# One level of Strassen for h, on 512-token blocks, with W_out streamed from DRAM

## What is computed

```python
scores = np.where(block_i >= block_j, q @ k.T / 8, -1e9)
x = softmax(scores) @ v                     # heads side by side: (2304, 512)
h = x @ moe_w_in                            # (2304, 2048)
x = (h * np.clip(h + 3.0, 0.0, 6.0) / 6.0) @ moe_w_out
h = x @ moe2_w_in
out = (h * np.tanh(np.log1p(np.exp(h)))) @ moe2_w_out
```

## Time and profile before

| what | us |
|---|---|
| median of 3 runs (lowest, highest) | 1022.93 (1021.42, 1024.57) |
| the profiled execution, whole | 1022.14 |
| its span, first to last instruction | 1020.3 |
| PE busy in the span | 995.0 |
| DVE, ACT, POOL busy | 662.3, 530.9, 279.7 |
| DMA moved | 78.89 MB, 77 GB/s over the span |

### The profile page before, as it was taken

How to read it: one execution, slowest core, us unless ns; L and a number is a source line. 1 busy time by engine, 2 the same in 40 slices (tenths; PEclk the granted TensorE clock), 3 DMA queues, 4 the chain that set the end, 5 groups by cost and what they waited for, 6 DMA issues and landing times.

```text
span 1020.3 us, 16901 instructions
## 1 busy us (share of the span) xinstructions
PE 995.0 (98%) x5700; PEld 931.1 (91%) x5700; DVE 662.3 (65%) x1280; ACT 530.9 (52%) x1161; POOL 279.7 (27%) x296
## 2 busy tenths in 40 slices
PE   6999999989999999999999999999999999999998
PEld 5888888889999999999999999999999999999996
DVE  5889889857332222222323559978888888888876
ACT  6889889846232222232323546555555465555553
POOL 7889889926022031130210200101001000010000
PEclk9999999989999999999999999999999999999999
DMA  6877886448121020120200342001000010000000
GB/s 156 238 184 212 212 208 169 101 142 257 39 73 52 20 81 23 54 69 0 88 28 31 132 140 75 24 1 48 16 31 23 8 39 23 0 31 0 32 1 31
DMA packets 42261, 78.89 MB, mean 77 GB/s; under 512 B 8032, under 2 KB 27616, under 8 KB 42208
## 3 DMA queue, kind: packets, MB, share of 16 engines
q1 hardware_dynamic: 36080, 68.48, 23.8%
q10 hardware_dynamic: 6128, 9.73, 2.6%
HBM read 59.24 MB, written 18.95 MB: 77 GB/s over the span
## 4 chain that ended last, share of the span: by engine, by line
PE 90%; DVE 4%; POOL 2%; issue 2%; ACT 1%; DMA 1%; SPq 0%; DVEq 0%; POOLq 0%
PE psum L525 38%; PE psum L500 13%; PE psum L502 13%; PE psum L501 13%; PE psum L451 4%; PE psum L430 4%; PE psum L406 3%; PE psum L411 3%; DMA qkin<-in_qk 0%; PE psum L409 0%; ACT prob L599 0%; POOL xraw L1002 0%; POOL xlo L1008 0%; DVE gsplit L845 0%; DVE wlo_early L832 0%
## 5 line engine op out<-in xcount | busy, mean ns | idle before, releaser
L1008 POOL TENSOR_TENSOR xlo<-xraw,xhi 128x384 f32 (+1 forms) x48 | 58.4, 1220 | 599.5 <-ACT xhi L659 599.5
L878 DVE SCALAR_TENSOR_TENSOR gbuf<-ebuf,psum 128x384 f32<-128x384 f32 x96 | 53.0, 552 | 218.3 <-ACT ebuf L711 218.3
L711 ACT ACTIVATE ebuf<-psum,three 128x384 f32<-128x384 f32 x96 | 55.7, 581 | 241.9 <-PE psum L502 241.9
L500 PE MATMUL psum<-xhi,whi_early 128*128 (+1 forms) x384 | 129.7, 338 | 1.3 <-POOL xlo L1008 1.3
L502 PE MATMUL psum<-xhi,wlo_early 128*128 (+1 forms) x384 | 129.4, 337 | 0.0
L501 PE MATMUL psum<-xlo,whi_early 128*128 (+1 forms) x384 | 129.2, 337 | 0.0
L502 PE MATMUL psum<-xhi,wlo_late 128*128 (+1 forms) x384 | 129.0, 336 | 0.0
L500 PE MATMUL psum<-xhi,whi_late 128*128 (+1 forms) x384 | 128.9, 336 | 0.0
L501 PE MATMUL psum<-xlo,whi_late 128*128 (+1 forms) x384 | 128.7, 335 | 0.0
L684 ACT ACTIVATE gsplit<-gbuf 128x384 fp32r<-128x384 f32 x192 | 100.1, 521 | 54.9 <-DVE gbuf L899 53.4
L845 DVE SCALAR_TENSOR_TENSOR gsplit<-gbuf,gsplit 128x384 fp32r<-128x384 f32 x192 | 123.0, 640 | 4.2 <-ACT gsplit L684 3.5
(11 more groups left out here) (89 smaller groups left out, 2298.2 us busy)
## 6 DMA issues: line engine op xcount, KB each, us to landing
wraw<-in_w SPq DMA_DIRECT2D x32, 512.0 KB, 3.5
qkin<-in_qk SPq DMA_DIRECT2D x43, 288.0 KB, 4.4
xraw<-attn_t SPq DMA_DIRECT2D x24, 384.0 KB, 3.3
attn_t<-late SPq DMA_DIRECT2D x44, 144.0 KB, 3.2
ystage<-in_qk SPq DMA_DIRECT2D x20, 288.0 KB, 4.5
xraw<-r_d SPq DMA_DIRECT2D x48, 96.0 KB, 3.3
x_t<-ystage ACTq DMA_DIRECT2D x24, 192.0 KB, 1.9
xraw<-x_t SPq DMA_DIRECT2D x24, 192.0 KB, 2.4
```

Source lines behind the costliest of these rows:

```text
L500: pe.matmul(bank(f % HB, TB), hi, x_part(xhi, blk, c), start=(c == 0), stop=False)
L711: nc.scalar.activation(ebuf[f % 2][:, :], bank(f % HB, TB), ACT.Relu, bias=three[:, 0:1]).then_inc(act_ready, 1)
L878: nc.vector.scalar_tensor_tensor(out=gbuf[f % 2][:, :], in0=e, scalar=6.0, in1=h, op0=ALU.min, op1=ALU.mult).then_inc(g_ready, 1)
L1008: nc.gpsimd.tensor_tensor(x_part(xlo, blk, c), xraw[c][:, 0, :], x_part(xhi, blk, c).bitcast(F32), ALU.subtract).then_inc(x_lo, 1)
```

## The change

**h by Strassen.** Blocks of tokens are now `plain` (256 tokens, the first of each layer) or full (512 tokens, four in each layer). The hidden dimension goes in 8 pairs of f; a `step` g is one pair in one block, 40 for each layer, 80 in all. For a full block, W_in's 512 x 256 piece and x's 512 x 512 block are cut in quarters, and the four quarters of h are made from 7 products instead of 8, in Winograd's form: with S1 = A21 + A22, S2 = S1 - A11, S3 = A11 - A21, S4 = A12 - S2 on the weights (DVE, `mix_w`) and T1 to T4 on x (POOL, `mix_x`). Each product is 2 chunks x 3 passes of 256 columns, in PSUM banks x, y, z. Sums that several quarters share are gathered in one bank and copied out on the way by ACT (`snap5`, `snap0`, `snap2`, `snap_3`); DVE adds the rest (`add_c11`, `add_c12`, `add_c22`). M4 may only start after snap3, M7 after snap2, M6 after snap0. For a plain block h stays an ordinary product, 24 matmuls of 256 columns for a pair.

**Order of PE.** The products of step s + 2 stand between the pieces of y of step s, one product and one piece in turn (`h_at`, `y_group`). In the full blocks of layer 0 y has 512 columns, not 384.

**Memory.** W_in's quarters A11, A12, A22 and S1 stay in SBUF (`whi`, `wlo`). S2 to S4 are split, stored to DRAM (`ext_d`, 0.79 MB a pair) and loaded again for each step of a full block (`ext`, two buffers). W_out is split f by f into one of `GS` = 3 slots (`osplit`) in the plain block, stored to `o_d` (`keep_o`, 0.52 MB an f), and loaded from there in the full blocks (`stream_o`). A slot may be filled anew when y of the f three before is done and its store has landed. In layer 0's plain block ACT makes the high part, in layer 1's POOL makes both. In layer 0 the weights of W_in are loaded twice, once for the quarters and once for S2 to S4 (`JOBS`), in steps -1 to 11; in layer 1 once, in steps 31 to 38. Loading, storing and y's stores are all in SP's queue.

**Mish.** e = exp(h), q = min((e + 1)^2, cap) + 1, r = exp(-ln q), and tanh(softplus(h)) = 1 - 2r. ACT makes the square; r gets one step of Newton's rule as before, folded into fewer products (`times_r`, `better_r`, `mish_times_h`).

The diff, cut:

```diff
-TB = 384
-NB = TOK // TB
+SQUARE_CAP = float(2 ** 28)
+TB = 512
+HT = TB // 2
+PAIRS = FT // 2
+NBL = 1 + (TOK - HT) // TB
+GS = 3
+PRODUCT_AT = {0: M2, 1: M5, 2: M1, 3: M3, 4: M6, 6: M7, 8: M4}
+JOBS = ([(0, p, True, False) for p in range(PAIRS)] + [(0, p, False, True) for p in range(PAIRS)] +
+        [(1, p, True, True) for p in range(PAIRS)])
...
@@ SP, after the attention
+            for s in range(-1, STEPS):
...
+                if s + 3 < STEPS and not plain((s + 3) // PAIRS):
+                    load_ext(s + 3)
+                if s > 0 and s % PAIRS == 0:
+                    store_y(s // PAIRS - 1)
+                if job_at(s + 1) is not None:
+                    load_w(job_at(s + 1))
+                if 0 <= s and 2 * s + 2 < 2 * STEPS and streamed(2 * s + 2):
+                    stream_o(2 * s + 2)
+                if 2 * s + 5 < 2 * STEPS and not streamed(2 * s + 5):
+                    load_o(2 * s + 5)
+                for i in (2 * s, 2 * s + 1):
+                    if i >= 0 and not streamed(i):
+                        keep_o(i)
+                blk = (s + 1) // PAIRS + 1
+                if (s + 1) % PAIRS == 0 and blk < NBLK:
+                    load_x(blk, 0)
+                blk = s // PAIRS + 1
+                if s % PAIRS == 2 and blk < NBLK and not plain(blk):
+                    load_x(blk, 1)
+                if 2 * s + 6 < 2 * STEPS and not streamed(2 * s + 6):
+                    load_o(2 * s + 6)
+                if 0 <= s and 2 * s + 3 < 2 * STEPS and streamed(2 * s + 3):
+                    stream_o(2 * s + 3)
+                if job_at(s) is not None and JOBS[job_at(s)][3]:
+                    store_ext(job_at(s))
...
@@ PE
...
+                    pe.wait_ge(snapped, SNAPS[g] + SNAP3 + 1)
+                    accumulate(x_bank(g), *resident(g, A22), g, T4, False, True).then_inc(product, 1)
+            for s in range(STEPS):
+                for k in range(9):
+                    if s + 2 < STEPS:
+                        h_at(s + 2, k)
+                    if k < 8:
+                        y_group(s, k)
...
@@ ACT
+            def split_o_hi(i):
+                act.wait_ge(o_loaded[i % GS], 16 * (i // GS + 1))
+                act.wait_ge(y_step, y_done(i - GS))
+                act.wait_ge(o_kept[i % GS], 16 * kept_before(i, i % GS))
+                nc.scalar.activation(osplit[i % GS][:, 0:D], oraw[i % GS][:, :], ACT.Copy).then_inc(first_o_hi, 1)
+            def mish_period(s):
...
+                    square(s + 1, 0)
+                    activate_h(s + 1, 1)
+                    square(s + 1, 1)
+                    split_g_hi(s, 1)
+                    snap5(s + 2)
+                    ln_d(s + 1, 0)
+                    snap0(s + 2)
+                    ln_d(s + 1, 1)
+                    exp_minus_ln(s + 1, 0)
+                    exp_minus_ln(s + 1, 1)
+                    snap2(s + 2)
+                next_x_hi(s, 0)
+                    activate_h(s + 2, 0)
+                    split_g_hi(s + 1, 0)
+                    snap_3(s + 2)
+                next_x_hi(s, 1)
...
@@ DVE
+            def mish_period(s):
...
+                    cap_square(s + 1, 0)
+                    mish_times_h(s, 1)
+                    cap_square(s + 1, 1)
+                    split_g_lo(s, 1)
+                    add_c11(s + 2)
+                    times_r(s + 1, 0)
+                    better_r(s + 1, 0)
+                    times_r(s + 1, 1)
+                    add_c12(s + 2)
+                    mish_times_h(s + 1, 0)
+                    better_r(s + 1, 1)
+                    split_g_lo(s + 1, 0)
+                    add_c22(s + 2)
...
@@ POOL
+            for s in range(-1, STEPS):
+                if GS <= 2 * s + 2 < 2 * STEPS and not streamed(2 * s + 2):
+                    split_o(2 * s + 2)
+                next_x(s)
+                if GS <= 2 * s + 3 < 2 * STEPS and not streamed(2 * s + 3):
+                    split_o(2 * s + 3)
```

1143 lines of the change are left out of this document (746 added, 397 removed).

## The result

The changed kernel took 1152.15 us in the median of 4 runs (1144.64 to 1157.62), the kernel before 1023.13 beside it (1021.42 to 1024.57): ratio 1.126, with a 95% interval of 1.119 to 1.132. Slower was forecast, but by 33 us and not by 129. The profiled execution has a span of 1149.5 us.

What follows compares the result with a forecast made beforehand. PE, busy 98% of the span, was taken as the bound. 1022.1 - 36.3 (PE) + 42 + 12 + 4 (transfers) + 8 (mish order) + 3 (tail) + 1 (attention) = 1056 us; range 1018 to 1092.

Steps and rivals of the forecast that it cites:

- layer 0's start: Layer 0's first steps: transfers and waits for W_out's slots, x and S2 to S4 cost +42 us (26 to 54).
- The short block of layer 1: Layer 1's first block: the slot loop of store, POOL's copy and subtraction, and load costs +12 us (4 to 20).
- PE's gain: Dense products on PE: h as 3072 matmuls of 256 columns at 118.4 ns; PE alone -36.3 us.
- rival (4): h on PE: a 256-column matmul costs 133 ns, so the gain is gone; 1100 us, chance 0.05.
- Layer 0's relu steps: Layer 0's full steps: ACT has 5.1 of 10.5 us, so they cost nothing.
- x's load: Layer 0's full blocks: the next x's second half stands before a stream PE wants, +4 us (0 to 8).
- (1): Transfers in layer 0's start and the short blocks: they hide, steps 0 to 12 lose 5 us; 1005 us, chance 0.13.
- (2): Layer 0's start: only the bound of 26 us holds, with smaller terms in layer 1; 1025 us, chance 0.11.
- sign for a wrong rate: First 130 us of the dense stage: a DMA rate over 360 GB/s would show the forecast wrong.
- The mish order: Layer 1's full steps: M4 waits 0.1 to 0.35 us for snap3 in each of 32 steps, +8 us (0 to 20).
- Rival (3): Layer 1's full steps: the mish chain closes on itself, steps take 11.5 us, 32 more; 1080 us, chance 0.14.
- The tail: The kernel's end: no h is left to cover the last pair's mish chain, so y(79) waits, +3 us.

Runs made afterwards that it cites:

- e1: The changed kernel with ACT's snap0 ahead of the high half of g for the step's second f in relu steps: 1141.55 us.
- e5: e1 with layer 1's weight splits moved behind the third snapshot and activation on ACT, and behind the last add on DVE: 1120.14 us.
- e6: The changed kernel with the load of x's second half behind W_out's second stream on SP, and x's work behind the second W_out split on POOL: 1173.01 us.
- e8: The changed kernel with the edits of e5, e6 and e7 together: 1093.89 us, ratio 1.067.
- e2: The changed kernel without the stores of split W_out, except the first f of each layer; loads keep number and size: 1132.86 us.
- e7: The changed kernel with each store of split W_out issued a step earlier, right behind the load that waits for the same low half: 1140.83 us.
- e15: e8 with W_out's low halves on DVE in layer 0's short block, and block 1's sum and scaling of x on only 8 columns: 1087.79 us.
- e9: e8 without the stores of split weights, except the first of each kind in each layer; loads keep number and size: 1072.92 us.
- e11: e8 with six extra additions on POOL, for which nobody waits, in each of steps 49 to 77: 1192.88 us.
- e10: e8 with POOL splitting only 64 of 512 columns of each W_out block in layer 1's short block: 1085.33 us.

## Why the prediction was wrong, step by step

Two steps of the sum failed most. The term for the order of ACT and DVE in layer 0's full steps was put at nothing: they lost 57 us, not 4. And layer 0's start was put at 42 us and lost 75. The short block of layer 1 added 17 to its 12.

**PE's gain: right.** The start-to-start distance of h's matmuls, profile after:

```profile
950.00 0.28 PE L703 MATMUL psum<-xhi,whi 128*128 128x256 f32 x1
950.12 0.28 PE L704 MATMUL psum<-xlo,whi 128*128 128x256 f32 x1
950.24 0.28 PE L705 MATMUL psum<-xhi,wlo 128*128 128x256 f32 x1
```

0.12 us, where 0.1184 was taken from the earlier trace rows; steps of 10.55, 8.40, 5.76 where nothing waits. So the -36.3 us are there to within 5 us, and rival (4) is out. (The lower bound of 27 doesn't follow from the rates named: 120 ns gives 33.)

**Layer 0's relu steps: the step that failed.** "Layer 0's relu steps have ACT at 5.1 of 10.5 and cost nothing" judged ACT by its sum. I walked the order for the mish (+8) and not for the relu, where one waiting split stands ahead of a snapshot. It cost 1.32 us in each full step that had nothing else (11.87 against 10.55); e1 gave 18.5 us back in steps 12 to 37. The same sentence named the weight splits as a risk and took them for covered: e5 gave back 11.1 more. x's load, forecast at 4, was 7.1 (e6). These three make 36.7 of the 57 us, and e8 has just these less (330.4 - 293.7). The other 20.7 are still in e8: 11 in steps 31 to 37, where M4 waits for `snap_3`; 6 in steps 12, 19 and 27, from waits of 1.0 to 4.2 us for a stream of `osplit` and the lower clock behind the longest; and 2.6 in steps 13, 21 and 29, where PE waits for x's low half, one of POOL's. The profile after has the same wait:

```profile
409.63 0.39 PE L703 MATMUL psum<-xhi,whi 128*128 128x256 f32 x1 [0.58 <-POOL xlo L1508]
```

No run tried these three.

**The start of layer 0: mechanism partly right, size wrong** (42 forecast, 75 measured). PE waits 6.4 us for `snap0` in steps 6 to 11 as well, but there e1 gave back nothing: another wait took its place. Right: the slots' loop (e2, e7), x ahead of splits in step 4. Wrong: the landings. I took 1.9 us of latency round the moving time, from a transfer alone. DMA issues of the profile after, from 218 to 386 us:

```profile
o_d<-osplit SPq DMA_DIRECT2D x16, 512.0 KB, 7.6
...
osplit<-o_d SPq DMA_DIRECT2D x10, 512.0 KB, 6.8
```

7.6 and 6.8 us in the median for 0.52 MB, against the 3.5 that the walk was built on (5.8 and 5.0 over the whole kernel). And x's first half was not in the walk as a transfer that POOL waits for in step 1, only in step 4: 18 us of idle POOL, then 5.1 of sums, then y's low half. Rivals (1) and (2) are out with 75. The rate was not what failed. A full queue moved 318 and 336 GB/s over 11 to 12 us in e15, and more in short stretches of the profile after, where PE had no work at all:

```profile
290.00:294.00 4.00, 0.00 (x0) 0.00 (x0) 0.43 (x2) 1.45 (x4) 0.75 (x1) 0.50 1.03 423
```

From 332 to 340 us it was 386. So the forecast's sign for a wrong rate, over 360, was there for some microseconds, and 346 was no ceiling. But from 225 to 386 us only 247 moved on average, since engines and queue waited for each other. A bound by bytes and a walk by latencies, each alone, were both too low. (The 42 were called the middle of 26 and 54, which is 40.)

**The clock: not in the sum at all.** Windows and PE's timeline, profile after:

```profile
230.00:238.00 8.00, 0.00 (x0) 0.02 (x1) 1.72 (x3) 2.89 (x6) 6.55 (x6) 0.54 0.62 234
238.00:242.00 4.00, 3.99 (x22) 4.00 (x23) 4.00 (x5) 1.60 (x4) 4.00 (x4) 0.63 0.80 225
```

```profile
269.33 0.55 PE L797 MATMUL psum<-ghi,osplit 128*128 128x256 f32 x1 [6.08 <-POOL osplit L1523]
...
270.75 0.41 PE L703 MATMUL psum<-xhi,whi 128*128 128x256 f32 x1
270.96 0.41 PE L704 MATMUL psum<-xlo,whi 128*128 128x256 f32 x1
271.17 0.41 PE L705 MATMUL psum<-xhi,wlo 128*128 128x256 f32 x1
```

The granted clock was at the lower level (1.2 GHz; 0.50 to 0.63 in these windows), and matmuls of 256 columns came 0.21 us apart instead of 0.12. The same is seen behind seven gaps of PE in steps 1 to 11, the shortest 3.0 us long and the longest 10.5. From 225 to 386 us some 100 distances lie at 0.19 to 0.225 us, and a few of 512 columns at 0.43 instead of 0.23: 11 us of PE in all. From 716 to 811 us it is some 40 and 15, 7 us. So such a gap of PE costs more than its length. Some of that PE time stands before a wait that would have been there anyway, so 11 us is a ceiling for what it added to the start.

**Layer 1's short block: mechanism right only in part** (12 forecast, 29 measured). I had the slots' loop set it. PE's waits from 716 to 811 us, profile after (us in total, times, longest):

```profile
PE psum L797 <- DVE glo L1289: 7.9, 6, 2.5
PE psum L797 <- POOL osplit L1523: 4.7, 2, 3.7
PE psum L703 <- POOL xlo L1508: 2.4, 1, 2.4
```

The longest sum is for g's low half on DVE; W_out's low half, the end of the loop, comes second, in steps 44 and 45. e7, which shortens the loop, gives back 4 us, and in e8 PE's waits for W_out are gone while 24 of the 29 us stay. The stores are 3 us of these (e9). What is left has DVE at up to twice its length beside a busy POOL: e11 shows that a busy POOL does this, and e10 gave back 10 us with less work on POOL, but doesn't tell how much by DVE. My own sum had POOL busy 47 of the block's 49 us; that this is also time in which DVE is held up was missing.

**The mish order: the size near, by luck.** The term was a wait of 0.1 to 0.35 us for M4 in each of 32 steps. Most full steps of layer 1 take 10.55 us, as layer 0's do in e1, and in them no matmul starts later than its predecessor's columns explain: the wait isn't there. The 5 us (8 forecast) come from steps with work on x or a copy of y, 10.7 to 11.15 us long; M4 waits 0.27 us in steps 51 and 59 only. Rival (3) is out here: no step of the changed kernel is over 11.2. With POOL busy (e11) M4 waits up to 4 us. The tail, profile after:

```profile
1138.93 0.73 PE L797 MATMUL psum<-osplit,ghi 128*128 128x512 f32 x2 [1.83 <-DVE glo L1289]
```

1.8 us of wait where the earlier trace rows had 0.3, and steps 78 and 79 take 13.6 us where 24 matmuls of 512 columns each make 11.1: 2.5, so +3 was right. The attention's end moved little in the profiled execution (step 0 at 218.8 us), and by up to 6 us in the variants (218.7 to 224.6); what does that wasn't looked into.

The small terms held in size. The three that failed were judged by a sum of busy time (the relu steps, POOL and DVE beside each other) or walked with the landing of a transfer alone (both short blocks, x), and all erred to the same side.

## What to carry to other kernels

Walk the order of every engine that another one waits for, in each kind of step, also where it is half idle: one waiting instruction ahead of a snapshot cost 1.3 us of every 10.5 us step on an engine busy 39% of the time (36.3 of 94 us). Before an experiment takes one wait away, look for a second that ends just ahead of it: in step 1 there were two within 1 us, and each of the runs that removed only one gained nothing there. When work is moved to a queue or an engine that was idle, ask who shares its landing time (loads behind stores) or its ports (DVE beside POOL). And where PE was full, a gap of some microseconds that a change opens can cost more than its length, as the matmuls behind it come at the lower clock.

## What the runs showed of the hardware that was not expected

- DVE's operations on 512 columns with all inputs in SBUF took 1.1 to 1.4 us instead of 0.5 to 0.85 beside a busy POOL; those that read PSUM stayed at 0.41 (e11). Six additions a step on POOL for which nothing waited cost 99 us.
- PE's clock was at the lower level behind seven gaps of 3.0 to 10.5 us in layer 0's start, and matmuls of 256 columns then came 0.21 us apart instead of 0.12.
- Issuing a store about one step earlier (e7) was worth 11 us with the same bytes. A transfer of 0.52 MB landed in 3.5 us in the kernel before and in 6.8 to 7.6 where loads and stores shared the queue.
- DMA moved 423 GB/s over 4 us and 386 over 8 us of the profile after, where the rows taken from the kernel before had 346 at best.
